# A channel MLP's first product by seven block products for eight, its weights loaded twice

## What is computed

```python
# _moe_ref: x [2, 768, 512], w_ch1 [512, 2048], w_ch2 [2048, 512]
xt = x.transpose(0, 2, 1)
h = xt @ U @ V
u = x + h.transpose(0, 2, 1)
ch = np.maximum(u @ w_ch1, 0.0) @ w_ch2
return (u + ch).astype(np.float32)
# _moe2_ref, on that
h = np.maximum(x @ w_in, 0.0)
u, v = (h[..., :d_ff // 2], h[..., d_ff // 2:])
v_n = (v - mu) / np.sqrt(var + 1e-06)
v_s = np.einsum('ts,bsd->btd', w_spatial, v_n) + b_spatial[None, :, None]
return ((u * v_s) @ w_out).astype(np.float32)
```

## Time and profile before

| | |
|---|---|
| three runs | 517.75 us median (517.63 to 517.79) |
| profiled execution | 517.66 us, of which the span on the core is 515.9 us |
| PE busy | 507.3 us, 98% of the span |
| DVE, ACT, POOL busy | 199.2, 182.2, 125.4 us |
| HBM read | 24.22 MB |

### The profile page before, as it was taken

The page is one execution under the profiler, slowest core; times in us unless marked ns, Lnnn a source line. Parts: engine busy times, 40 slices in busy tenths (PEclk is TensorE's granted clock), DMA queues, the critical chain, the costliest instruction groups (busy, mean ns, idle before and its releaser), DMA issues.

```text
span 515.9 us, 7643 instructions
## 1 busy us (share of the span) xinstructions
PE 507.3 (98%) x2870; PEld 422.7 (82%) x2870; DVE 199.2 (39%) x556; ACT 182.2 (35%) x452; POOL 125.4 (24%) x122
## 2 busy tenths in 40 slices
PE   8999999999999999999999999999999999999997
PEld 7787677787888888888888888888888998889995
DVE  5887688511233522221113211112564256540440
ACT  7888688532322310210101333223343213331121
POOL 6795755353344300000000252431000000000000
PEclk9999999999999999999999999999999999999999
DMA  8811800132222300000000123230000000110002
GB/s 248 278 47 41 286 4 2 44 110 94 81 83 81 112 12 1 0 1 0 1 0 1 42 71 93 61 113 0 2 0 0 1 2 20 42 41 22 1 22 102
DMA packets 12246, 27.88 MB, mean 54 GB/s; under 512 B 2224, under 2 KB 2224, under 8 KB 12208
## 3 DMA queue, kind: packets, MB, share of 16 engines
q1 hardware_dynamic: 10336, 23.96, 14.4%
q10 hardware_dynamic: 1872, 3.41, 1.8%
HBM read 24.22 MB, written 3.15 MB: 53 GB/s over the span
## 4 chain that ended last, share of the span: by engine, by line
PE 93%; ACT 3%; DVE 2%; issue 1%; DMA 1%; SPq 0%; ACTq 0%; DVEq 0%
PE bank L1040 29%; PE bank L1252 25%; PE bank L1171 25%; PE bank L1093 4%; PE bank L1075 3%; PE bank L1060 3%; ACT prob L829 2%; PE bank L1111 1%; PE bank L1116 1%; DMA qk_raw<-in_qk 1%; DVE prob L528 1%; PE bank L1141 1%; PE bank L1130 1%; ACT bias L817 0%; DVE probT L539 0%
## 5 line engine op out<-in xcount | busy, mean ns | idle before, releaser
L1252 PE MATMUL bank<-hid,w_slot 128*128 128x512 f32 x576 | 139.2, 390 | 0.0
L1171 PE MATMUL bank<-u_split,w_slot 128*128 128x512 f32 x576 | 138.7, 390 | 0.0
L1252 PEld LDWEIGHTS bank<-hid,w_slot 128*128 128x128 f32 x576 | 107.7, 188 | 23.2 <-issue 0.9
L1171 PEld LDWEIGHTS bank<-u_split,w_slot 128*128 128x128 f32 x576 | 107.7, 188 | 22.5 <-issue 0.2
L695 DVE SCALAR_TENSOR_TENSOR hid<-bank,hid 128x512 fp32r<-128x512 f32 x48 | 33.2, 692 | 186.8 <-ACT hid L933 186.6
L933 ACT ACTIVATE hid<-bank 128x512 fp32r<-128x512 f32 x48 | 28.7, 599 | 202.0 <-PE bank L1171 202.0
L829 ACT ACTIVATE prob<-prob,row_min 128x256 f32<-128x256 f32 (+1 forms) x96 | 46.0, 480 | 13.6 <-DVE row_min L528 13.5
L1040 PE MATMUL bank<-sp_slot,vn 128*128 128x384 f32 x288 | 50.3, 334 | 0.0
L1040 PEld LDWEIGHTS bank<-sp_slot,vn 128*128 128x128 f32 x288 | 50.0, 188 | 0.2
L428 POOL TENSOR_TENSOR w_slot<-stage,w_slot 128x1024 fp32r<-128x1024 f32 x14 | 33.5, 2394 | 48.0 <-ACT w_slot L883 48.0
L428 POOL TENSOR_TENSOR in_slot<-stage,in_slot 128x1024 fp32r<-128x1024 f32 x4 | 9.6, 2393 | 121.5 <-ACT in_slot L883 121.5
(11 more groups left out here) (94 smaller groups left out, 506.6 us busy)
## 6 DMA issues: line engine op xcount, KB each, us to landing
stage<-in_w_ch SPq DMA_DIRECT2D x16, 512.0 KB, 3.3
...
stage<-in_w_in SPq DMA_DIRECT2D x4, 512.0 KB, 3.2
stage<-in_w_out SPq DMA_DIRECT2D x2, 512.0 KB, 3.5
...
```

Source lines behind the costliest of these rows:

```text
L1171: last = mm(h_bank[g % 2][:], w_slot[f][:, a, k * P:(k + 1) * P], u_split[c][:, m, k, :], start=(k == 0 and p == 0), stop=(k == KD - 1 and ...
L1252: last = mm(c_ring[(KD * c + k) % 6][:], w_slot[f][:, a, 512 + k * P:512 + (k + 1) * P], hid[g % 2][:, m, :], start=(f == 0 and a == HI an ...
```

## The change

Chunk 0 goes as before. Chunks 1 and 2 are taken together, and so are hidden blocks 2i and 2i+1, a pair (i = 0 to 7). The first product of a pair is then a 2x2 matrix of blocks (r: which hidden block; n: which chunk), each a sum over two halves of the features. Eight block products of 6 matmuls would make it. The change makes it with seven, after Strassen and Winograd: four of them use sums of weight blocks (S1 to S4, made by POOL, `sum_pair`) or of token blocks (T1 to T4, made once by DVE, `sum_tokens`), and the results are put together afterwards. `seven` (PE) makes blocks x = 0 to 6 in four banks: 0, then 2 on top of it, in bank 6; 1 in bank 7; 3, then 5, in bank 4; 4, then 6 on top, in bank 5. ACT copies block 0 out before block 2 is added (`first_sb`), DVE adds the others up in SBUF (`add_part`, three `part` buffers), ACT and DVE round and split the four hidden blocks (`high_block`, `low_block`, `hid2`).

`contract_pair` then makes the second product, in two halves: n = 0 (chunk 1) and n = 1 (chunk 2), each 24 matmuls onto the same four banks, and after each half DVE adds each bank to `uT` (`sum_y`, released by `pair_acc` bank by bank). So `sum_y` runs 4 + 64 times where it ran 12 times.

SBUF no longer holds all the weights: six `w_slot` places in a ring, and w_ch is loaded twice (`LOADS`, 44 loads where there were 28). The buffers' places change with it, those of `in_slot`, `sp_slot`, `out_slot`, `y_split` and the gate among them, and so does the point at which w_in, w_spatial and w_out are staged. The last eight mixes, two each at g = 6 to 9 before, now stand four each at f = 6 and 7, in two alternating banks (`mix_bank`). DVE's `sum_tokens` comes at f = 8, and the seven operands of the block products are rounded and split at f = 8 to 15.

```diff
-        w_slot = [at(f"w_slot{f}", [P, 2, 1024], F32R, SLOT * f) for f in range(FT)]
+        RING = (0, 1, 2, 12, 13, 14)
+        w_slot = [at(f"w_slot{m}", [P, 2, 1024], F32R, SLOT * RING[m % 6]) for m in range(2 * FT)]
+        s_slot = [at(f"s_slot{r}", [P, 2, 4, 2 * P], F32R, SLOT * (15, 11)[r]) for r in range(2)]
+        u_op = [at(f"u_op{j}", [P, 2, 2, CT], F32R, SLOT * (3 + j)) for j in range(7)]
+        s_raw = [at(f"s_raw{r}", [P, 4, 2 * P], F32, SLOT * (15, 11)[r] + 4096) for r in range(2)]
+        u_raw = [at(f"u_raw{j}", [P, 2, CT], F32, SLOT * (3 + j) + 4096) for j in range(7)]
+        part = [at(f"part{r}", [P, CT], F32, SLOT * 10 + 2048 * r) for r in range(3)]
...
-        h_bank = bank[4:6]
-        c_ring = [bank[i] for i in (0, 1, 2, 3, 6, 7)]
-        g_ring = [bank[i] for i in (0, 1, 4, 5, 2, 3, 6, 7)]
+        h_bank, c_bank = bank[4:6], bank[0:4]
+        seven_bank = [bank[i] for i in (6, 7, 4, 5)]
+        g_ring = [bank[i] for i in (6, 7, 4, 5, 0, 1, 2, 3)]
...
+        SEVEN = (((0, 0), 0, 0, False), ("S2", 1, 1, False), ((0, 1), 2, 0, True), ("S3", 3, 2, False),
+                 ("S1", 4, 3, False), ((1, 1), 5, 2, True), ("S4", 6, 3, True))
+        SUMS = {"S1": 0, "S2": 1, "S3": 2, "S4": 3}
+        B11, T2, B21, T3, T1, T4, B22 = range(7)
+        BLOCKS = ((0, 0), (1, 1), (1, 0), (0, 1))
...
+                    if kind2 == "w" and m >= FT:
+                        sp.wait_ge(s_sum, 4 * ((m - FT) // 2) + 4)
...
+            def sum_pair(i, n):
+                w0, w1 = stage[(n - 1) % 2], stage[n % 2]
+                near_half, far_half = slice(0, 2 * P), slice(2 * P, 4 * P)
...
+                pool.wait_ge(stage_in[(n - 1) % 2], 16 * ((n - 1) // 2 + 1))
+                pool.wait_ge(stage_in[n % 2], 16 * (n // 2 + 1))
...
+                else:
+                    pool.wait_ge(seven_ps, 7 * (i - 1))
+                nc.gpsimd.tensor_tensor(dst("S1"), w1[:, near_half], w1[:, far_half], ALU.add).then_inc(s_sum, 1)
+                nc.gpsimd.tensor_tensor(dst("S3"), w0[:, near_half], w1[:, near_half],
+                                        ALU.subtract).then_inc(s_sum, 1)
+                pool.wait_ge(s_sum, 4 * i + 1)
+                nc.gpsimd.tensor_tensor(dst("S2"), dst("S1"), w0[:, near_half], ALU.subtract).then_inc(s_sum, 1)
+                pool.wait_ge(s_sum, 4 * i + 3)
+                nc.gpsimd.tensor_tensor(dst("S4"), w0[:, far_half], dst("S2"), ALU.subtract).then_inc(s_sum, 1)
+            def split_sums(i):
+                sums = s_slot[i % 2]
+                pool.wait_ge(s_hi, i + 1)
+                nc.gpsimd.tensor_tensor(sums[:, LO, :, :], s_raw[i % 2][:],
+                                        sums[:, HI, :, :].bitcast(F32), ALU.subtract).then_inc(s_lo, 1)
...
+            def sum_tokens():
+                def low(j, k):
+                    return u_raw[j][:, k, :]
+                def u(c, k):
+                    return uT[:, k, c * CT:(c + 1) * CT]
+                for k in range(2):
+                    vec.tensor_tensor(low(T1, k), u(2, k), u(1, k), ALU.subtract).then_inc(t_sum, 1)
+                for k in range(2):
+                    dve.wait_ge(t_sum, k + 1)
+                    vec.tensor_tensor(low(T2, k), u(2, 2 + k), low(T1, k), ALU.subtract).then_inc(t_sum, 1)
+                for k in range(2):
+                    vec.tensor_tensor(low(T3, k), u(2, 2 + k), u(2, k), ALU.subtract).then_inc(t_sum, 1)
+                for k in range(2):
+                    dve.wait_ge(t_sum, 2 + k + 1)
+                    vec.tensor_tensor(low(T4, k), u(1, 2 + k), low(T2, k), ALU.subtract).then_inc(t_sum, 1)
...
+            def split_op(j):
+                for k in range(2):
+                    dve.wait_ge(u_hi, KD + 2 * j + k + 1)
+                    vec.tensor_tensor(u_op[j][:, LO, k, :], raw_op(j, k), u_op[j][:, HI, k, :].bitcast(F32),
+                                      ALU.subtract).then_inc(u_lo, 1)
...
                 y = uT[:, k, c * CT:(c + 1) * CT]
-                dve.wait_ge(c_acc, FT * (c + 1))
-                vec.tensor_tensor(y, c_ring[j % 6][:], y, ALU.add).then_inc(y_sum, 1)
+                if e < KD:
+                    dve.wait_ge(c_acc, FT)
+                else:
+                    dve.wait_ge(pair_acc, e - KD + 1)
+                vec.tensor_tensor(y, c_bank[k][:], y, ALU.add).then_inc(y_sum, 1)
...
+            def low_block(i, x):
+                r, n = BLOCKS[x]
+                src = (seven_bank[0], part[1], part[2], part[0])[x]
+                dve.wait_ge(hid2_hi, 4 * i + x + 1)
+                vec.scalar_tensor_tensor(hid2[r][n][:, LO, :], src[:], 0.0, hid2[r][n][:, HI, :].bitcast(F32),
+                                         ALU.max, ALU.subtract).then_inc(hid2_lo, 1)
+            def add_part(i, dst, src, held, products, after):
+                dve.wait_ge(seven_ps, 7 * i + products)
+                if after:
+                    dve.wait_ge(part_sum, 5 * i + after)
+                vec.tensor_tensor(part[dst][:], part[src][:], seven_bank[held][:], ALU.add).then_inc(part_sum, 1)
+            for i in range(PAIRS):
+                dve.wait_ge(first_sb, i + 1)
+                add_part(i, 0, 0, 1, 2, 0)
+                low_block(i, 0)
+                add_part(i, 1, 0, 2, 4, 1)
+                if i == 0:
+                    sum_y(0)
+                    sum_y(1)
+                add_part(i, 1, 1, 3, 5, 2)
+                if i == 0:
+                    sum_y(2)
+                    sum_y(3)
+                add_part(i, 2, 0, 2, 6, 1)
+                low_block(i, 1)
+                low_block(i, 2)
+                add_part(i, 0, 0, 3, 7, 1)
+                low_block(i, 3)
+                for x in range(2 * KD):
+                    if i == PAIRS - 1 and x == KD:
+                        for k in range(KD):
+                            split_y(k)
+                    sum_y(KD + 2 * KD * i + x)
+            for j in range(KD, CH * KD):
+                split_y(j)
...
+                if kind == "w":
+                    if 3 <= k < 6:
+                        act.wait_ge(pv_done, QUADS)
+                    elif 6 <= k < FT + 6:
+                        act.wait_ge(c_acc, k - 5)
+                    elif k >= FT + 6:
...
+            for i in range(PAIRS):
+                act.wait_ge(seven_ps, 7 * i + 1)
+                sc.activation(part[0][:], seven_bank[0][:], ACT.Copy).then_inc(first_sb, 1)
+                if i == 0:
+                    split_stage(FT + 2)
+                high_block(i, 0)
+                if i == 0:
+                    split_stage(FT + 3)
+                elif i < PAIRS - 1:
+                    round_sums(i + 1)
+                high_block(i, 1)
+                high_block(i, 2)
+                high_block(i, 3)
+                if i == 0:
+                    round_sums(1)
+                if i == 2:
+                    split_stage(load_no("in", 0))
+                    split_stage(load_no("in", 1))
+                if i < PAIRS - 2:
+                    for m in range(FT + 2 * i + 4, FT + 2 * i + 6):
+                        split_stage(load_no("w", m))
+                if i == PAIRS - 2:
+                    split_stage(load_no("in", 2))
+                    split_stage(load_no("sp", 0))
+                    split_stage(load_no("sp", 5))
...
+            for k in range(KD):
+                round_y(k)
+            split_stage(load_no("in", 3))
+            for s in range(1, 5):
+                split_stage(load_no("sp", s))
+            for k in range(KD):
+                round_y(KD + k)
...
+            def seven(i, first, end):
+                w = (w_slot[FT + 2 * i], w_slot[FT + 2 * i + 1])
+                for x in range(first, end):
+                    block, op, held, more = SEVEN[x]
+                    if x == 0:
+                        pe.wait_ge(w_lo, load_no("w", FT + 2 * i + 1) + 1)
+                    if x == 1:
+                        pe.wait_ge(s_lo, i + 1)
+                    if x == 2:
+                        pe.wait_ge(first_sb, i + 1)
+                    if x == 5:
+                        pe.wait_ge(part_sum, 5 * i + 2)
+                    if x == 6:
+                        pe.wait_ge(part_sum, 5 * i + 3)
+                    if i == 0:
+                        pe.wait_ge(u_lo, KD + 2 * op + 2)
+                    for k in range(2):
+                        for p, (a, m) in enumerate(PASSES):
+                            if block in SUMS:
+                                lhs = s_slot[i % 2][:, a, SUMS[block], k * P:(k + 1) * P]
+                            else:
+                                r, half = block
+                                lhs = w[r][:, a, (2 * half + k) * P:(2 * half + k + 1) * P]
+                            last = mm(seven_bank[held][:], lhs, u_op[op][:, m, k, :],
+                                      start=not more and k == 0 and p == 0, stop=k == 1 and p == 2,
+                                      skip_group_check=True)
```

(35 more changed lines are left out.)

360 lines of the change are left out of this document (175 added, 185 removed).

## The result

| | before | after |
|---|---|---|
| median of the runs | 517.73 us (517.63 to 517.79) | 510.98 us (510.94 to 511.02) |
| span of the profiled execution | 515.9 us | 508.9 us |
| HBM read | 24.22 MB | 32.61 MB |

The change makes the kernel faster by 6.75 us: ratio 0.987, 95% interval 0.9853 to 0.9887. The forecast was 511.0 us.

What follows compares the result with a forecast made beforehand. The prediction took PE (TensorE), busy 507.3 of 515.9 us, to bound the kernel: 517.66 - 10.9 (48 matmuls fewer) + 4.0 (waits in the second product) + 0.2 = 511.0 us, range 507.0 to 516.0.

Steps and rivals of the forecast that it cites:

- What goes: First product of chunks 1 and 2: 336 matmuls instead of 384, 48 x 0.2266 = 10.9 us off PE.
- Where PE waits: Second product, start of half n = 1: PE waits for DVE's bank sums, 0.5 us per pair, 4.0 in all.
- Bank 3: Second product, half n = 1: DVE's sum ends at 15.85, PE is due at 15.64; cost 0.41 us per pair.
- The 0.08 for bank 2: Second product, half n = 1: bank 2 free at 15.17, weight load due 15.19; cost about 0.08 us per pair.
- The seam: Passage from the last pair to the gated part: DVE's split of y's first chunk among POOL's splits, 0.1 us late.
- It ends 0.1 us late: DVE's split of y's first chunk, among POOL's splits of in_slot 3 and sp_slot 1, before the gated part.
- Edits costed at nothing: Token sums, operand splits, weight staging, mixes, pair weight sums: taken as covered by slack, so no PE time.
- Token sums: Last half of chunk 0: eight DVE sums, 5.4 us, plus one POOL hold of at most 2.4; low half ready at 9.4.
- The sum: Whole kernel: 517.66 - 10.9 + 4.0 + 0.2 = 511.0 us.
- Rival 1: Pairs: POOL's split holds DVE's SBUF-only low halves, 2.7 us per pair, 21.8 in all, 528.6 us; chance 0.11.
- Rival 2: Pairs: sums drain sooner than laid out and no PE wait is seen, 506.8 to 508.3 us; chance 0.10.
- Rival 3: Blocks 2, 5 and 6: spares of 0.25 to 0.3 us fail too, 513.2 to 516.6 us; chance 0.15.

## Why the prediction was right

- **What goes.** 48 x 0.2266 = 10.9 us. Confirmed: 10.95 when they are put back.
- **Where PE waits.** Place, number and cause stood as predicted: eight stops, half n = 1, DVE's fourth sum. Bank 3 was laid out at 0.41 us and cost 0.40: from PE's start of the half (226.26) to DVE's end (227.15) are 0.89 us, as worked out. The 0.08 for bank 2 did not come; its sum ends just ahead of its weight load. So the term is 3.2 us and not 4.0, and the period 20.80 and not 20.9.
- **The seam.** "It ends 0.1 us late" was the mis-sized step: the splits made PE lose 0.62. The prediction names both POOL splits but shows no working for the 0.1, so how many holds it allowed for stays open. The row shows two holds in succession, and the kernel with the added wait shows that without the second, PE does not stop.
- **Edits costed at nothing.** Token sums, operand splits, twice-loaded weights, the ring and the mixes: no new wait of PE in chunk 0 and none at L1481; the 0.10 us of the books is there before chunk 0 starts. One cover was thinner than laid out. The token sums were priced with one POOL hold, 7.8 us; they took 9.3 (148.42 to 157.73), two of the eight being held (2.90 and 2.88 us, at 149.02 and 154.85):

```profile
148.42 3.49 DVE L748 TENSOR_TENSOR u_raw<-uT 128x512 f32<-128x512 f32 x2
...
154.25 3.48 DVE L756 TENSOR_TENSOR u_raw<-uT,u_raw 128x512 f32<-128x512 f32 x2
157.65 0.68 DVE L782 SCALAR_TENSOR_TENSOR hid<-bank,hid 128x512 fp32r<-128x512 f32 x1
```

The low half behind them was ready 11.35 us after its predecessor's product ended (158.33 - 146.98), not 9.4, and PE asked at 12.7: 1.3 us of spare, not 3.3. The added load traffic (8.4 MB) shows nowhere in PE's waits.
- **The sum.** 4.0 + 0.2 was forecast for what comes back, and 3.2 + 0.62 + 0.10 = 3.9 came inside the span. Another 0.2 us came outside it: 2.0 us of the profiled execution lie there (510.94 - 508.9), where it was 1.8, and no step of the prediction covers that. So the agreement to 0.1 us is partly luck: the banks were 0.8 too dear, the seam 0.4 too cheap (with the whole 0.2 put down to it), and the remaining 0.3 unpriced.
- **Rival 1 (POOL's hold).** The mechanism is real here: 526.7 us, slower than before, when POOL's splits begin 4.6 us earlier (219.41, against 224.04 in the change as made). It stayed away for the reason given, the order in which ACT releases POOL (low halves at 731 ns). Its price, 2.7 us per pair, rested on a hold through one split of 2.39 us (15.06 + 0.56), and one instruction at a time is what the traces show. No run brought the last low half the 0.97 us late that it was priced for, so the 2.7 itself is not measured; with all three low halves under POOL, a pair lost 3.1. The Trainium skill, "SBUF — State Buffer", section "Who interferes with whom", has the exclusive hold for one instruction, whichever engine starts first; the traces agree both ways, now for POOL too: its split at the seam took 2.29 us beside 1.86 for the next of the same shape.
- **Rival 2 (no wait).** Wrong for the change as made. Without the two stops the kernel takes 506.87 us, where the prediction worked out 506.8 for PE without waits. Of the 4.0 us between the two spans, 3.2 and 0.6 are the two stops; the last 0.2 lies ahead of the pairs, which begin at 187.61 there and at 187.78 in the change as made, and no edit acts there.
- **Rival 3 (thin spares).** The spare of block 2 is as laid out (0.29), and handoffs ran no longer than bare durations. Blocks 5 and 6 were not tried; they show no wait.
